# Turning v and the output by 32x32 blocks on VectorE, with x made channel-major, in a fused attention and feed-forward kernel

## The reference

```python
q, k, v: (1, 6016, 256) f32
qn = q / (norm(q, axis=1) + 1e-6);  kn = k / (norm(k, axis=1) + 1e-6)   # norms over all tokens
a = softmax(kn.T @ qn / tau)                                            # 256 x 256
x = v @ a                                                               # 6016 x 256
xn = x / sqrt(mean(x * x, axis=-1) + 1e-6) * rms_g
g = xn @ w_gate;  val = xn @ w_val                                      # 256 -> 1536
y = (g / (1 + exp(-g)) * val) @ w_out                                   # 1536 -> 256
h = y @ w_in2                                                           # 256 -> 2048
out = (h - tanh(h)) @ w_out2                                            # 2048 -> 256
```

## Time and profile before

| what | value |
| --- | --- |
| median of 3 runs | 1258.31 us (1258.27 to 1258.67) |
| profiled execution: span from the first to the last instruction | 1259.6 us |
| mean granted TensorE clock | 0.992 |
| TensorE / VectorE / ScalarE busy | 97% / 68% / 30% |
| first product of the first tile starts at | 77.35 us |
| starts of tiles 1 to 11 | 165.57, 264.65, 363.94, 463.23, ..., 1158.29 us |
| last product starts at | 1253.78 us |
| sigmoid or tanh of 512 columns on ScalarE (L476), mean | 599 ns |
| reciprocal of 4 columns on VectorE (L553), mean | 171 ns |

### The profile page before, as it was taken

How to read it: one execution, slowest core, us unless ns; L and a number is a source line. 1 busy time by engine, 2 the same in 40 slices (tenths; PEclk the granted TensorE clock), 3 DMA queues, 4 the chain that set the end, 5 groups by cost and what they waited for, 6 DMA issues and landing times.

```text
span 1259.6 us, 16669 instructions
## 1 busy us (share of the span) xinstructions
PE 1227.1 (97%) x5715; PEld 1023.9 (81%) x5715; DVE 862.1 (68%) x1390; ACT 377.0 (30%) x645; POOL 68.1 (5%) x38
## 2 busy tenths in 40 slices
PE   6889999999999999999999999999999999999998
PEld 5679888888888888888888888888888888888877
DVE  7978965766766766667676676586576676666665
ACT  6552421421421331321321232142142132133121
POOL 5533300000000000000000000000000000000000
PEclk9889999999999999999999999999999999999999
DMA  7633000000000000000000000000000000000000
GB/s 262 227 121 113 1 13 18 1 1 34 1 0 33 0 0 33 0 0 33 0 1 17 17 0 17 17 0 17 17 0 0 33 0 0 17 0 0 17 1 17
DMA packets 16875, 33.91 MB, mean 27 GB/s; under 512 B 1872, under 2 KB 8528, under 8 KB 16848
## 3 DMA queue, kind: packets, MB, share of 16 engines
q1 hardware_dynamic: 16704, 33.30, 7.7%
q10 hardware_dynamic: 144, 0.26, 0.1%
HBM read 27.40 MB, written 6.16 MB: 27 GB/s over the span
## 4 chain that ended last, share of the span: by engine, by line
PE 91%; DVE 5%; issue 2%; ACT 1%; DMA 0%; SPq 0%; DVEq 0%; ACTq 0%
PE ring L800 50%; PE out_acc L813 20%; PE y_acc L813 15%; PE ring L762 3%; DVE out_rows L526 2%; DVE h_hi L659 1%; PE ring L785 1%; PE ring L746 1%; PE ring L773 1%; DMA qk_in<-in_q_dram 0%; PE y_acc L725 0%; DVE act L670 0%; DVE act L692 0%; DVE qk_lo L521 0%; PE y_acc L730 0%
## 5 line engine op out<-in xcount | busy, mean ns | idle before, releaser
L476 ACT ACTIVATE act<-ring 128x512 f32<-128x512 f32 (+1 forms) x336 | 198.4, 590 | 700.8 <-PE ring L800 694.8
L661 DVE TENSOR_TENSOR h_lo<-act,h_hi 128x512 fp32r<-128x512 f32 (+1 forms) x336 | 233.3, 694 | 11.6
L800 PE MATMUL ring<-x_hi,we_hi 128*128 128x512 f32 (+1 forms) x576 | 229.0, 398 | 4.6 <-DVE act L670 3.2
L800 PE MATMUL ring<-x_hi,we_lo 128*128 128x512 f32 (+1 forms) x576 | 227.3, 395 | 0.0
L800 PE MATMUL ring<-x_lo,we_hi 128*128 128x512 f32 (+1 forms) x576 | 226.8, 394 | 0.0
L670 DVE TENSOR_TENSOR act<-ring,act 128x512 f32<-128x512 f32 (+1 forms) x144 | 97.9, 680 | 178.6 <-ACT act L476 177.7
L692 DVE TENSOR_TENSOR act<-ring,act 128x512 f32<-128x512 f32 (+1 forms) x192 | 130.1, 677 | 97.8 <-ACT act L476 96.7
L659 DVE CAST h_hi<-act 128x512 fp32r<-128x512 f32 (+1 forms) x336 | 157.4, 468 | 13.8
L813 PE MATMUL out_acc<-h_hi,wl_hi 128*128 128x512 f32 (+1 forms) x384 | 148.1, 386 | 2.4 <-DVE h_lo L661 2.3
L800 PE MATMUL ring<-y_hi,wl_hi 128*128 128x512 f32 (+1 forms) x384 | 149.0, 388 | 1.2 <-DVE y_lo L682 0.9
L800 PE MATMUL ring<-y_hi,wl_lo 128*128 128x512 f32 (+1 forms) x384 | 148.0, 385 | 0.0
(11 more groups left out here) (100 smaller groups left out, 1265.6 us busy)
## 6 DMA issues: line engine op xcount, KB each, us to landing
qk_in<-in_k_dram SPq DMA_DIRECT2D x15, 384.0 KB, 3.8
qk_in<-in_q_dram SPq DMA_DIRECT2D x15, 384.0 KB, 4.7
v_in<-in_v_dram SPq DMA_DIRECT2D x11, 512.0 KB, 3.3
out_dram<-out_rows SPq DMA_DIRECT2D x10, 512.0 KB, 2.6
w_in<-in_moe_w_out_dram SPq DMA_DIRECT2D x14, 256.0 KB, 3.0
w_in<-in_moe_w_in_dram SPq DMA_DIRECT2D x8, 256.0 KB, 3.2
w_in<-in_moe_w_gate_dram SPq DMA_DIRECT2D x6, 256.0 KB, 4.2
w_in<-in_moe_w_val_dram SPq DMA_DIRECT2D x6, 256.0 KB, 4.9
```

Source lines behind the costliest of these rows:

```text
L476: nc.scalar.activation(act[:, u % RING, 0:width], b.bank(name)[:, 0:width], func).then_inc(act_ready, 1)
L661: nc.vector.tensor_tensor(h_lo[:, slot, 0:width], act[:, slot, 0:width], f32(h_hi[:, slot, 0:width]), ALU.subtract).then_inc(h_ready, 1)
L800: ins = nc.tensor.matmul(b.bank(name)[:, 0:width], weights(c, w_part), (hi if part else lo)[:, c, 0:width], start=c == 0 and w_part and pa ...
```

## The change

**Turnings.** TensorE turns nothing more. v is loaded by eight DMAs a tile (one for each half of the channels and each 32 partitions), each of 32x16 runs of 32 numbers (128 bytes), so that every block of 32x32 stands where its turned block belongs; VectorE's 32x32 transpose then turns all blocks in one instruction (`turn_v`, behind unit 4), ScalarE casts the high part (behind unit 5), VectorE makes the low part (`split_v`, behind unit 7). The output is turned by VectorE straight out of `out_acc` (`turn_out`, one half behind each of the units 0 and 1 of the next tile) and stored by eight DMAs of the same kind.

**x.** `make_x` has `a` as weights and `vt` moving: 12 products of 512 columns into `out_acc`, channels along the partitions. ScalarE squares and copies each half (`take_x`). VectorE adds the two squared halves, turns the sum by blocks and reduces over 32 columns (behind hidden units 0, 1, 2); TensorE multiplies the 16 columns with `quads`, a matrix that adds the four groups of 32 partitions and spreads the sum (`add_quads`, behind hidden unit 4); ScalarE takes the root; VectorE takes the reciprocal and turns it, spread, back to columns (behind 6), scales x by it and `rms_g` (7 and 8), ScalarE casts (9 and 10), VectorE makes `x_lo` (10 and 11). GpSimd builds `quads` at the start in seven more mask steps, and TensorE's first product waits for all of them.

**Tiles and buffers.** The short tile is now last: 11 tiles of 512, then 384. `w_in` has three stages. The buffers are laid out anew. Worked out from the programs' buffer sizes (SBUF byte addresses within a partition; each buffer is a multiple of 32 bytes), with the distance past a multiple of 64:

| operand | before | past 64 | after | past 64 |
| --- | --- | --- | --- | --- |
| `a_hi` | 2304 | 0 | 2688 | 0 |
| `vt_hi` | 10496 | 0 | 14976 | 0 |
| `x_hi` | 22784 | 0 | 27264 | 0 |
| `h_hi` | 39264 | 32 | 45696 | 0 |
| `y_hi` | 55648 | 32 | 62080 | 0 |
| `we_hi` | 88416 | 32 | 86656 | 0 |
| `wl_hi` | 162400 | 32 | 160384 | 0 |

The low parts stand as the high ones do. `ident` stood at 1152 and `x_rows` at 18688.

The diff, cut to the new functions and where they are called; the old turnings, their calls and their ring banks go:

```diff
+SQ = 32
+QUADS = P // SQ
...
+V_TURN_AT, V_SPLIT_AT = 4, 7
+SUM_AT = 4
+SQRT_AT = 5
+X_ADD, X_TURN, X_REDUCE, X_RMS, X_SCALE, X_CAST, X_SPLIT = 0, 1, 2, 6, 7, 9, 10
...
+    WSTAGES = 3
...
+    def tokens(rows, t, width, half, quad):
+        part = rows[t * TILE:t * TILE + width, :] if isinstance(t, int) else rows[bass.ds(t * TILE, width), :]
+        at = half * P + quad * SQ
+        return part[:, at:at + SQ].rearrange("(b r) c -> r b c", r=SQ)
     def block_parts(b):
...
+        quads = sb("quads", [P, P], F32)
...
+        vt = sb("vt", [P, KC, TILE], F32)
...
+        xt = sb("xt", [P, KC, TILE], F32)
...
+        out_rows = sb("out_rows", [P, KC, TILE // SQ, SQ], F32)
...
+            def load_v(t, width):
+                if not (isinstance(t, int) and t == 0):
+                    sp.wait_ge(v_turned, t)
+                for half in range(KC):
+                    for quad in range(QUADS):
+                        sp.dma_start(v_in[quad * SQ:(quad + 1) * SQ, half, 0:width // SQ, :],
+                                     tokens(v_rows, t, width, half, quad)).then_inc(v_loaded, 16)
             def load_block(n):
...
+            def store(t, width):
+                for half in range(KC):
+                    sp.wait_ge(out_turned, t * KC + half + 1)
+                    for quad in range(QUADS):
+                        sp.dma_start(tokens(out, t, width, half, quad),
+                                     out_rows[quad * SQ:(quad + 1) * SQ, half, 0:width // SQ, :]).then_inc(stored, 16)
...
+                pool.wait_ge(constants, 6 + n)
+                nc.gpsimd.affine_select(out=quads[:], in_=quads[:], compare_op=ALU.not_equal, fill=1.0,
+                                        base=(n - (QUADS - 1)) * SQ, pattern=[[-1, P]],
+                                        channel_multiplier=1).then_inc(constants, 1)
+            pool.wait_ge(constants, CONSTANTS)
...
+            def cast_v(t, width):
+                act_e.wait_ge(v_turned, t + 1)
+                nc.scalar.copy(vt_hi[:, :, 0:width], vt[:, :, 0:width]).then_inc(vt_hi_ready, 1)
...
+            def take_x(t, width):
+                for d in range(KC):
+                    act_e.wait_ge(x_full, t * KC + d + 1)
+                    nc.scalar.activation(squares[:, d, 0:width], x_acc[:, d, 0:width],
+                                         ACT.Square).then_inc(sq_ready, 1)
+                    nc.scalar.copy(xt[:, d, 0:width], x_acc[:, d, 0:width]).then_inc(x_copied, 1)
+            def root(t, width):
+                act_e.wait_ge(sums_full, t + 1)
+                nc.scalar.activation(rms[:, 0:width // SQ], token_sums[:, 0:width // SQ], ACT.Sqrt,
                                      scale=1.0 / C, bias=eps[:, 0:1]).then_inc(rms_ready, 1)
...
+            def cast_x(t, width, c):
+                act_e.wait_ge(xn_ready, t * KC + c + 1)
+                nc.scalar.copy(x_hi[:, c, 0:width], xt[:, c, 0:width]).then_inc(x_hi_ready, 1)
             for i in range(2):
...
+                    if f == V_TURN_AT + 1 and not last:
+                        cast_v(t + 1, ahead)
                 for d in range(KC):
                     wait_sum(act_e, t, d, y_full, G)
                     nc.scalar.copy(y_hi[:, d, 0:width], y_acc[:, d, 0:width]).then_inc(y_hi_ready, 1)
+                if not last:
+                    take_x(t + 1, ahead)
...
+                        if f == SQRT_AT:
+                            root(t + 1, ahead)
+                            nc.scalar.activation(warm[:, :], eps[:, :], ACT.Sigmoid)
+                        if X_CAST <= f < X_CAST + KC:
+                            cast_x(t + 1, ahead, f - X_CAST)
...
+            def turn_v(t, width):
+                dve.wait_ge(v_loaded, t * TILE_DMAS + TILE_DMAS)
+                nc.vector.transpose(vt[:, :, 0:width].rearrange("p k (b r) -> p k b r", r=SQ),
+                                    v_in[:, :, 0:width // SQ, :]).then_inc(v_turned, 1)
...
+            def split_v(t, width):
+                dve.wait_ge(vt_hi_ready, t + 1)
+                nc.vector.tensor_tensor(vt_lo[:, :, 0:width], vt[:, :, 0:width], f32(vt_hi[:, :, 0:width]),
+                                        ALU.subtract).then_inc(vt_ready, 1)
...
+            def add_squares(t, width):
+                dve.wait_ge(sq_ready, t * KC + KC)
+                nc.vector.tensor_tensor(squares[:, 0, 0:width], squares[:, 0, 0:width], squares[:, 1, 0:width],
+                                        ALU.add).then_inc(sum_step, 1)
+            def turn_squares(t, width):
+                dve.wait_ge(sum_step, t * SUM_STEPS + 1)
+                nc.vector.transpose(turned_sum[:, 0:width], squares[:, 0, 0:width]).then_inc(sum_step, 1)
+            def reduce_squares(t, width):
+                dve.wait_ge(sum_step, t * SUM_STEPS + 2)
+                nc.vector.tensor_reduce(sums[:, 0:width // SQ],
+                                        turned_sum[:, 0:width].rearrange("p (b r) -> p b r", r=SQ),
+                                        AX_X, ALU.add).then_inc(sum_step, 1)
+            def spread_scales(t, width):
                 dve.wait_ge(rms_ready, t + 1)
...
+                nc.vector.reciprocal(rrms[:, 0:width // SQ], rms[:, 0:width // SQ]).then_inc(scale_step, 1)
+                dve.wait_ge(scale_step, t * SCALE_STEPS + 1)
+                nc.vector.transpose(scales[:, 0:width].rearrange("p (b r) -> p b r", r=SQ),
+                                    rrms[:, 0:width // SQ].unsqueeze(2).to_broadcast([P, width // SQ, SQ])
+                                    ).then_inc(scale_step, 1)
+            def scale_x(t, width, c):
+                dve.wait_ge(scale_step, t * SCALE_STEPS + SCALE_STEPS)
+                dve.wait_ge(x_copied, t * KC + c + 1)
+                nc.vector.scalar_tensor_tensor(
+                    out=xt[:, c, 0:width], in0=xt[:, c, 0:width], scalar=g_c[:, c:c + 1],
+                    in1=scales[:, 0:width], op0=ALU.mult, op1=ALU.mult).then_inc(xn_ready, 1)
+            def split_x(t, width, c):
+                dve.wait_ge(x_hi_ready, t * KC + c + 1)
+                nc.vector.tensor_tensor(x_lo[:, c, 0:width], xt[:, c, 0:width], f32(x_hi[:, c, 0:width]),
+                                        ALU.subtract).then_inc(x_ready, 1)
+            def turn_out(t, width, d):
+                wait_sum(dve, t, d, out_full, U)
+                if d == 0 and not (isinstance(t, int) and t == 0):
+                    dve.wait_ge(stored, t * TILE_DMAS)
+                nc.vector.transpose(
+                    out_rows[:, d, 0:width // SQ, :],
+                    out_acc[:, d, 0:width].rearrange("p (b r) -> p b r", r=SQ)).then_inc(out_turned, 1)
...
+                    if f < KC and not first:
+                        turn_out(t - 1, TILE, f)
+                    if f == V_TURN_AT and not last:
+                        turn_v(t + 1, ahead)
+                    if f == V_SPLIT_AT and not last:
+                        split_v(t + 1, ahead)
...
+                        if f == X_ADD:
+                            add_squares(t + 1, ahead)
+                        if f == X_TURN:
+                            turn_squares(t + 1, ahead)
+                        if f == X_REDUCE:
+                            reduce_squares(t + 1, ahead)
+                        if f == X_RMS:
+                            spread_scales(t + 1, ahead)
+                        if X_SCALE <= f < X_SCALE + KC:
+                            scale_x(t + 1, ahead, f - X_SCALE)
+                        if X_SPLIT <= f < X_SPLIT + KC:
+                            split_x(t + 1, ahead, f - X_SPLIT)
...
+            for d in range(KC):
+                turn_out(TILES - 1, SHORT, d)
...
+            def make_x(t, width):
+                pe.wait_ge(vt_ready, t + 1)
+                for d in range(KC):
...
+                        for a_part, v_part in PASSES:
+                            ins = nc.tensor.matmul(x_acc[:, d, 0:width],
+                                                   (a_hi if a_part else a_lo)[:, c, d * P:(d + 1) * P],
+                                                   (vt_hi if v_part else vt_lo)[:, c, 0:width],
+                                                   start=c == 0 and a_part and v_part,
+                                                   stop=c == KC - 1 and not a_part)
+                    ins.then_inc(x_full, 1)
+            def add_quads(t, width):
+                pe.wait_ge(sum_step, t * SUM_STEPS + SUM_STEPS)
+                nc.tensor.matmul(token_sums[:, 0:width // SQ], quads[:, :], sums[:, 0:width // SQ],
+                                 start=True, stop=True).then_inc(sums_full, 1)
...
                 if not last:
-                    make_x(t + 1, b, TILE)
+                    if not first:
+                        pe.wait_ge(out_turned, t * KC)
+                    make_x(t + 1, ahead)
...
+                        if f == LAG:
+                            if not last:
```

(5 more changed lines are left out.)

402 lines of the change are left out of this document (118 added, 284 removed).

## The result

The changed kernel takes **1225.8 us** (median of four runs, 1223.6 to 1228.3) against 1258.5 for the kernel before: 0.974 of its time, 95% interval 0.972 to 0.976. The forecast was 1222, with 1209 to 1244 as its range. The profiled run took 1223.6 us and its span is 1221.8, 37.8 less than before's 1259.6.

What follows compares the result with a forecast made beforehand. TensorE, without idle time in a middle tile, was taken as the bound. 83.4 + 103.5 + 10 x 95.85 - 0.6 + 71.7 + 7 = 1223.5 us of span, less 1.3, gave 1222; range 1209 to 1244.

Steps and rivals of the forecast that it cites:

- The sum: Whole kernel: start, first tile, ten middle tiles, last tile and end make 1223.5 us, against a span of 1259.6.
- The turnings: Middle tile: 24 turnings in three groups of 8 leave TensorE, 0.88 us a group, 2.6 us a tile.
- The distances: Middle tile: operands at equal phases past 64 bytes bring 144 x products from 234.4 to 226.7 ns, 1.1 us.
- (a): Rival, middle tile: phase has nothing to do with it, x stays at 234.4 ns; 1237 us; chance 0.16.
- (b): Rival, middle tile: a moving operand on a multiple of 64 is slow, all steps 234.4 ns; 1258 us; chance 0.06.
- (e): Rival, all products: the 13 ns go too once all is aligned, a tile of 90.3 us; 1157 us; chance 0.04.
- The wait: Middle tile, 16-column product: TensorE waits about 0.45 us for VectorE's third extra operation, 0.2 to 1.0 us.
- The start: Up to the first x product: 77.35 - 0.6 + 0.56 + 2.1 + 0.5 + 3.5 = 83.4 us.
- (c): Rival, start and end: a 128-byte run costs about 60 ns of an engine, v's 15 us; 1238 us; chance 0.11.
- (d): Rival, every tile: from 194 ns a run the queue bounds, kernel slower; 1574 us at 250 ns; chance 0.05.
- The first tile: First tile, now 512 wide: 103.5 us, with 2.6 for 13 cold steps and 5 (0 to 12) for stalls.
- The last tile and the end: Last tile 71.7 us, 408 x 173.3 ns plus 1.0 of waiting; end 7 us (6 to 13) after the last product.

Runs made afterwards that it cites:

- the aligned kernel before: The kernel before with 32 bytes of padding ahead of its act buffer, nothing else: 1257.6 us, 0.998 of before.
- the last run: Changed kernel, 16-column product one hidden unit later, tile 0's v loaded behind the last piece, quads built behind the pieces, last four stores by ScalarE: 1213.95 us.

## Why the prediction was right, and where it was not

**The bound.** TensorE has no idle time in a middle tile, before or after, so the tile is its steps: right. The forecast for a tile missed by 0.15 us in 95.7.

**The sum** stood at 1223.5 us of span, and the forecast took 1.3 off it, because the span of before lay that much above its median. But every time on record is 1.8 us above its span (1223.6 and 1221.8), so the sum stood for 1225.3, and 1225.8 was measured: most of the 3.8 us between forecast and result is this conversion, from an execution of before that was longer than its median.

**The turnings**: 2.6 forecast, 2.72 measured by putting them back.

**The distances.** "Equal phases run at columns plus 13, unequal ones slower" holds; that the phase is taken from a multiple of 64 bytes, the step on which the table of addresses was read, is wrong. By that step the aligned kernel before would have gained 14 us and gained 1.6. The forecast came out by luck in this term: the changed layout happens to put all operands at 128 past a multiple of 256 too. The size, 1.3 a tile, was 1.18 where x of the old kernel was moved, and 1.27 where x of the changed one was put 32 off. Rivals (a), (b) and (e) fell with the 226.7 ns of all products in the changed kernel.

**The wait**: 0.45 forecast (0.40 by its own terms, 9.92 less 9.52), 0.14 measured, below the 0.2 to 1.0 that was to be its sign. The turning was sized rightly (705 ns for 0.69); the sum took three units at 1.79 us and three extras at 0.72, 7.53 in all, and they took 7.2 (529.09 to 536.26 in the trace). The product itself was put at 0.11 and takes 0.25. The two misses partly cancel: wait, product and slow step were to cost 0.65 and cost 0.48, which is the tile's miss. What the prediction left out is the clock: moved one unit earlier, the wait cost 2.7 to 5.7 us a tile.

**The start**: 83.4 forecast, 81.9 measured (81.2 to 85.6 over nine traces). The load of v with its mask steps and the turning was to cost 3.4 and cost 1.4 up to the making of x, though between 1 and 5 over the nine traces. Its eight issues were to add 2.6 us to SP's queue and added 4.3 (4.61 instead of 0.34). The chain of x was to cost 2.1 and cost 2.6. Rival (c), 60 ns a run, is out at 11 to 13, and tile 0's v landed 6.6 us after its first issue; (d) is out with it.

**The first tile**: 103.5 forecast, 106.0 measured, within its bounds of 0 to 12 us for stalls. Waits make 5.7 us of it (5 taken), products at the lower clock 4.5 (2.6 taken, for 13 products). One wait makes about 4.2 us of both, 2.6 beyond what it costs in a middle tile and 1.6 of slow products behind it, and the last run, without it, is 4.1 us shorter here. The prediction had priced that wait for middle tiles only: the 16-column product starts 2.9 us behind the product ahead, since VectorE's reduction stands behind a cast that takes 1.64 us beside GpSimd's subtraction of weights, and the clock falls behind the wait.

```profile
147.94 2.39 POOL L379 TENSOR_TENSOR wl_lo<-w_in,wl_hi 128x1024 fp32r<-128x1024 f32 x1 [2.53 <-ACT wl_hi L407]
...
148.97 1.64 DVE L665 CAST h_hi<-act 128x512 fp32r<-128x512 f32 x1
...
151.98 0.48 PE L764 MATMUL y_acc<-sums,quads 128*128 128x16 f32 x2 [2.52 <-DVE sums L545]
...
152.00:155.00 3.00, 3.00 (x8) 0.53 0.00 0
```

**The last tile and the end**: 71.7 and 7 forecast, 71.64 and 6.05 measured. The last issue starts 3.90 us after the last product (3.85 forecast) and lands 1.8 us later (2.4 or more assumed); 3.85 and 2.4 are 6.25, and the 7 holds 0.75 that no term names.

```profile
1215.76 0.34 PE L791 MATMUL out_acc<-h_hi,wl_lo 128*128 128x384 f32 x1
1216.23 3.90 SPq L309 DMA_DIRECT2D out_dram<-out_rows  x8
```

## What to carry to other kernels

When TensorE is busy without a gap, compare the step from start to start between products of the same shape: a kind that is 3% slower than another is worth a look at where its operands start, and moving x by 96 bytes brought 1% here. Small turnings that interrupt a stream of products cost their columns and a slow product behind them, and VectorE takes them over at the price of a copy. A short product whose input comes off another engine belongs one unit later than where it just fits: of ten missed handovers of 2.3 to 2.9 us here, nine cost more than their length.

## What was not expected of the hardware

- A product of 512 columns in f32r steps at 226.7 ns when moving operand and weights start at the same distance past a multiple of 256 bytes, and at 233 to 234.4 for five of the six other distances tried; one took 229.4. Why is open.
- Behind a wait of 2.9 us (2.3 in one tile) TensorE ran products at the lower clock in nine tiles of ten, mostly 8 or 13 of them, and none in the tenth.
- One product of 16 columns in f32 is two instructions and takes 0.25 us behind a short wait, 0.14 without one, besides the slow step behind it.
- Eight loads with 4,096 runs of 128 bytes held SP's queue for 4.5 to 6.9 us, and the next piece landed 1.5 to 5.6 us later than behind one load in long runs. A run took an engine 11 to 13 ns.
